# One core: attention, routed experts and a dense block. Keys read in place, logits per token, tile-by-tile scatter of expert rows

## The reference, cut to what matters

```python
# attention: B=2, H=8, S=768, D=64; blocks of 32 keys are summarised
k_sum = k.reshape(B, H, 24, 32, D).max(axis=3)
v_sum = v.reshape(B, H, 24, 32, D).mean(axis=3)
scores_l = scale * q @ k.T            # kept where |i - j| < 16, else -1e9
scores_s = scale * q @ k_sum.T + log(32)
a = softmax(concat([scores_l, scores_s]))
x = (a @ concat([v, v_sum])).reshape(1536, 512)      # token-major
# experts: w_gate (512, 8), w1 (8, 512, 1024), w2 (8, 1024, 512)
do_compute = x @ w_skip > 0
e_idx, gate_w = argmax(x @ w_gate), softmax(x @ w_gate)[e_idx]
x[do_compute] += gate_w * (relu(x @ w1[e_idx]) @ w2[e_idx])
# dense: w_in (512, 2048), w_out (2048, 512)
h = x @ w_in
out = (h * cos(h)) @ w_out
```

## Time and profile before

| | |
|---|---|
| median of 3 runs | 599.25 us (594.43 to 600.09) |
| profiled execution | 601.41 us, span 599.7 us |
| attention, to the first instruction of the routing | 0 to 152.5 us |
| routing, to the first expert product | 152.5 to 178.9 us |
| experts, to the last second product | 178.9 to 299.2 us |
| to the first dense matmul | 299.2 to 316.5 us |
| dense | 316.5 to 599.7 us |
| busy: PE, DVE, ACT, POOL | 494.9, 314.7, 217.7, 128.5 us |

### The profile page before, as it was taken

How to read it: one execution, slowest core, us unless ns; L and a number is a source line. 1 busy time by engine, 2 the same in 40 slices (tenths; PEclk the granted TensorE clock), 3 DMA queues, 4 the chain that set the end, 5 groups by cost and what they waited for, 6 DMA issues and landing times.

```text
span 599.7 us, 10654 instructions
## 1 busy us (share of the span) xinstructions
PE 494.9 (83%) x4077; PEld 384.2 (64%) x4077; DVE 314.7 (52%) x582; ACT 217.7 (36%) x522; POOL 128.5 (21%) x139
## 2 busy tenths in 40 slices
PE   2876666597168788968788988899999999999997
PEld 1665555453165456546476766678888888888885
DVE  4475565441601112111064898886777676766764
ACT  1354444363001010101062645544544444544443
POOL 6357555431033100000063313430000000000000
PEclk9978787798579889889798999999999999999999
DMA  6837888756999807077742000020400000100001
GB/s 170 208 114 230 242 263 261 210 139 204 373 404 372 323 16 290 17 304 281 292 117 99 1 0 0 2 70 2 141 0 1 1 1 0 72 0 1 1 1 70
DMA packets 48938, 79.32 MB, mean 132 GB/s; under 512 B 4345, under 2 KB 30969, under 8 KB 48890
## 3 DMA queue, kind: packets, MB, share of 16 engines
q1 hardware_dynamic: 44434, 70.68, 35.5%
q0 software_dynamic: 2080, 6.82, 3.5%
q10 hardware_dynamic: 2376, 1.18, 0.7%
HBM read 65.95 MB, written 11.14 MB: 129 GB/s over the span
## 4 chain that ended last, share of the span: by engine, by line
PE 54%; DMA 19%; DVE 11%; issue 6%; ACT 4%; SPq 3%; POOL 2%; ACTq 1%; DVEq 0%; POOLq 0%
PE bank L1133 11%; PE bank L1135 11%; PE bank L1134 11%; DMA rows_sorted<-y_out 10%; DMA v_tok<-v_pairs 5%; PE bank L1161 3%; PE bank L1058 3%; PE bank L1020 3%; PE bank L1174 3%; DVE turns L947 3%; DMA x_plain<-x_stage 2%; PE bank L1041 2%; DVE reduced L951 2%; DVE reduced L954 2%; PE bank L1140 1%
## 5 line engine op out<-in xcount | busy, mean ns | idle before, releaser
L1133 PE MATMUL bank<-wout_hi,gT_hi 128*128 128x512 f32 x192 | 76.0, 396 | 9.8 <-DVE gT_lo L966 9.8
L1133 PE MATMUL bank<-x2T,win_hi 128*128 128x512 f32 x192 | 76.4, 398 | 1.4 <-DVE x2T L934 1.4
L1134 PE MATMUL bank<-x2T,win_hi 128*128 128x512 f32 x192 | 75.3, 392 | 0.0
L1135 PE MATMUL bank<-x2T,win_lo 128*128 128x512 f32 x192 | 75.3, 392 | 0.0
L1135 PE MATMUL bank<-wout_hi,gT_lo 128*128 128x512 f32 x192 | 74.8, 390 | 0.0
L1134 PE MATMUL bank<-wout_lo,gT_hi 128*128 128x512 f32 x192 | 74.8, 390 | 0.0
L679 ACT ACTIVATE turns<-reduced,half_pi 128x512 f32<-128x512 f32 x48 | 34.7, 723 | 86.5 <-DVE reduced L957 86.5
L947 DVE TENSOR_SCALAR turns<-turns 128x512 f32<-128x512 f32 x48 | 33.0, 687 | 58.1 <-ACT turns L672 58.1
L672 ACT ACTIVATE turns<-bank,quarter 128x512 f32<-128x512 f32 x48 | 32.9, 686 | 59.1 <-PE bank L1135 59.1
L890 DVE COPY y_out<-bank 128x128 f32 x18 | 5.2, 292 | 90.8 <-PE bank L1174 57.0
L1133 PEld LDWEIGHTS bank<-wout_hi,gT_hi 128*128 128x128 f32 x192 | 36.0, 188 | 21.6 <-DVE gT_lo L966 14.4
(11 more groups left out here) (155 smaller groups left out, 863.7 us busy)
## 6 DMA issues: line engine op xcount, KB each, us to landing
w_slot<-weights SPq DMA_DIRECT2D x80, 512.0 KB, 7.0
rows_sorted<-zeros SPq DMA_DIRECT2D x7, 512.0 KB
k_padded<-k_T SPq DMA_DIRECT2D x8, 384.0 KB, 7.3
q_raw<-q_T SPq DMA_DIRECT2D x8, 384.0 KB, 4.8
v_tok<-v_pairs SPq DMA_DIRECT2D x8, 384.0 KB, 5.2
v_window<-v_pairs SPq DMA_DIRECT2D x8, 384.0 KB, 4.3
x_plain<-x_stage SPq DMA_DIRECT2D x8, 384.0 KB, 7.8
x_tile<-x_plain SPq DMA_DIRECT2D x12, 256.0 KB
```

The lines of the kernel that those rows point to most:

```text
L1133: te.matmul(out_ap, a[0], b[0], start=start, stop=False)
L1134: te.matmul(out_ap, a[0], b[1], start=False, stop=False)
L1135: return te.matmul(out_ap, a[1], b[0], start=False, stop=stop)
```

## The change

- Attention: `keys` is gone. PE multiplies each query tile by the 32 summary columns (`ksum`, L975 after) and by 96 columns of the padded keys in place (L976 after), two matmuls where there was one. `v_tok` and `q_raw` have two buffers, `k_padded` three, and SP loads them before the windows of the pair before. `place_q` works on a third of a pair behind each `normalise`; the first pair is placed by DVE. `copy_x` writes straight into `xT`; the block sums move to the head of `values`, and their copy from ACT to DVE.
- Logits: in each `transpose_x` PE adds the x block's product with the gate weights, tokens along the partitions, into one bank that collects all 12 token tiles. The stage's end has no logits matmuls, copies or transposes left.
- x is kept whole in `x_tok`: one store of half of x beside pair 5, the rest at the end. The six zero blocks are stored after the last pair's weights.
- Routing: fewer and shorter DVE steps, two of the products on ACT and POOL, and the one-hot matrix made in two halves. Added: the scatter rows, spread over four column groups by four small matmuls.
- Experts: all copies of a tile are on ACT, in one loop. POOL, once its 14 gathers are through, scatters each tile's y rows to their tokens with an indirect transfer (L517 after). `copy_y` waits for `y_free`, which POOL counts up in that same program; there are four y slots. Every four scatters use four semaphores, so a scatter waits for the one four back. SP loads expert 2's weights at the end of the attention, and two chunks of experts 3 and 4 behind each of the first eight blocks that have landed. DVE splits `w_in` during the last experts. `y` is loaded in order by SP.
- Dense: ACT makes the high part of `w_out` (two chunks ahead, six in the first group's slots 2 to 7), POOL all eight low parts. Nothing else changes.

```diff
+SLOT_OF = (0, 1, 3, 4, 2, 0, 1, 3)
...
             def load_k(i):
-                sp.dma_start(kpad[i % 2][:, WINDOW:WINDOW + S], kT[i, :, :]).then_inc(k_loaded[i % 2], 16)
+                ge(sp, scores_ready, GPP * (i - 2))
+                sp.dma_start(kpad[i % 3][:, WINDOW:WINDOW + S], kT[i, :, :]).then_inc(k_loaded[i % 3], 16)
             def load_q(i):
-                ge(sp, q_placed, i)
-                sp.dma_start(qraw[:, :], qT[i, :, :]).then_inc(q_loaded, 16)
+                ge(sp, q0_placed, min(i - 1, 1))
+                ge(sp, q_placed, GPP * (i - 2))
+                sp.dma_start(qraw[i % 2][:, :], qT[i, :, :]).then_inc(q_loaded[i % 2], 16)
             def load_vtok(i):
-                ge(sp, vs_ready, i)
-                sp.dma_start(vtok[:, :, :], v2[i, :, :].rearrange("(t p) d -> p t d", p=P)).then_inc(vtok_loaded, 16)
+                ge(sp, vs_ready, i - 1)
+                sp.dma_start(vtok[i % 2][:, :, :], v2[i, :, :].rearrange("(p t) d -> p t d", t=TPB))\
+                    .then_inc(vtok_loaded[i % 2], 16)
...
             for i in range(PAIRS):
-                sp.wait_ge(keys_ready, i + 1)
+                if i > 0 and i + 2 < PAIRS:
+                    load_k(i + 2)
                 if i + 2 < PAIRS:
-                    load_k(i + 2)
                     load_q(i + 2)
+                    load_vtok(i + 2)
                 if i > 0:
                     sp.wait_ge(xps_ready, GPP * i)
                 if i + 1 < PAIRS:
                     load_windows(i + 1)
                     place_vsum(i + 1)
-                if i + 2 < PAIRS:
-                    load_vtok(i + 2)
                 for n in range(BESIDE * i, BESIDE * (i + 1)):
                     load_chunk(n // NCH, n // NCH, n % NCH)
-                if i > 0:
-                    store_zeros(i - 1)
-                if i > 1:
-                    store_x(i - 2)
-            store_x(PAIRS - 2)
-            store_x(PAIRS - 1)
-            sp.wait_ge(xt_copied, STEPS)
-            sp.wait_ge(zero_stored, 16 * PAIRS)
-            for e in range(BESIDE, SLOTS):
-                for c in range(NCH):
-                    load_chunk(e, e, c)
+                if i == PPB + 1:
+                    store_x(GPP * PPB, 0, TPB, 0, PPB)
+            store_x(GPP * (PAIRS - 2), TPB, NT, 0, PPB - 2)
+            sp.wait_ge(zeros_ready, 1)
+            for k in range(NT // 2):
+                dst = yd[CG * P * (2 * k + NBLK):CG * P * (2 * k + NBLK + 2), :].rearrange("(p r) f -> p (r f)", p=P)
+                sp.dma_start(dst, zeros[:, :]).then_inc(zero_stored, 16)
+            store_x(GPP * (PAIRS - 1), TPB, NT, PPB - 2, PPB - 1)
+            for gr in range(GPP):
+                store_x(STEPS - GPP + gr + 1, TPB + 2 * gr, TPB + 2 * gr + 2, PPB - 1, PPB)
+            sp.wait_ge(xps_ready, STEPS)
+            for c in range(NCH):
+                load_chunk(2, SLOT_OF[2], c)
+            for k in range(NCH):
+                sp.wait_ge(blocks_ready, k + 1)
+                if k == NCH // 2:
+                    sp.wait_ge(x_stored, 16 * XSTORES)
+                    sp.wait_ge(zero_stored, 16 * (NT // 2))
+                for c in (2 * k, 2 * k + 1):
+                    load_chunk(3 + c // NCH, SLOT_OF[3 + c // NCH], c % NCH)
...
-            for done, src, s in ((1, 5, 0), (2, 6, 1), (3, 7, 2), (4, E, 3), (6, E + 1, 0)):
+            for done, src, s in ((1, 5, 0), (2, 6, 1), (3, 7, 3), (4, E, 4), (6, E + 1, 0)):
                 sp.wait_ge(expert_done, done)
                 for c in range(NCH):
                     load_chunk(src, s, c)
+            sp.wait_ge(y_all, 1)
+            for q in range(TPG):
+                load_y(q, q)
...
+            def place_q(s):
+                i, gr = s // GPP, s % GPP
+                pool.wait_ge(q_loaded[i % 2], 16 * (i // 2) + 16)
+                ge(pool, scores_ready, s - 2 * GPP + 1)
+                src = qraw[i % 2][:, GT * QT * gr:GT * QT * (gr + 1)].rearrange("p (t q) -> p t q", q=QT)
+                dst = qbd[i % 2][:, GT * gr:GT * (gr + 1), :]
+                g.tensor_scalar(dst[:, :, 0:QT], src, head_mask[:, 0:1], None, ALU.mult)
+                g.tensor_scalar(dst[:, :, QT:2 * QT], src, head_mask[:, 1:2], None, ALU.mult).then_inc(q_placed, 1)
...
+            pool.wait_ge(base_ready, 2)
+            nblocks = pool.value_load(base[0:1, E + 1:E + 2], min_val=E // CG, max_val=NBLK)
+            pool.wait_ge(idx4_ready, 1)
+            pool.wait_ge(zero_stored, 16 * (NT // 2))
+            def scatter_block(k):
+                for j in range(CG):
+                    ge(pool, y_stored[j], 16 * k)
+                    g.tensor_copy(idx_now[:, j:j + 1], idx4[:, bass.ds(k, 1), j:j + 1].rearrange("p o q -> p (o q)"))\
+                        .then_inc(idx_copied, 1)
+                    pool.sem_inc(y_free, 1)
+                    pool.wait_ge(idx_copied, CG * k + (j + 1))
+                    primed(pool, y_copied, CG * k + (j + 1))
+                    pool.sem_inc(y_taken, 1)
+                    pool.indirect_dma_start(yd, bass.IndirectOffsetOnAxis(ap=idx_now[:, j:j + 1].bitcast(U32), axis=0),
+                                            y_out[:, j, :], None).then_inc(y_stored[j], 16)
+            scatter_block(0)
+            with pool.Fori(1, nblocks) as k:
+                scatter_block(k)
+            for j in range(CG):
+                pool.wait_ge(y_stored[j], 16 * nblocks)
+            pool.sem_inc(y_all, 1)
+            for c in range(NCH):
+                pool.wait_ge(wout_hi_done, c + 1)
+                g.tensor_tensor(wout_lo[:, c, :], wslot[0][:, c, :], wout_hi[:, c, :].bitcast(F32), ALU.subtract)\
+                    .then_inc(wout_lo_done, 1)
...
+            def copy_block(n):
+                act.wait_ge(blocks_ready, n // CG + 1)
+                primed(act, t1_ready, n)
+                sc.activation(xblk[:, :], xg[:, bass.ds(n // CG, 1), :].rearrange("p o f -> p (o f)"), ACT.Copy)\
+                    .then_inc(block_copied, 1)
...
+            def copy_y(n):
+                primed(act, y_ready, n)
+                act.wait_ge(y_free, n)
+                sc.activation(y_out[:, bass.ds((n - 1) % CG, 1), :].rearrange("p o f -> p (o f)"), y_ps[:, 0:P], ACT.Copy)\
+                    .then_inc(y_copied, 1)
+            def copy_hT(n):
+                primed(act, t2_ready, n + 1)
+                primed(act, y_ready, n)
+                sc.activation(hT[:, :, :], ht_ps[:, 0:JC * P].rearrange("p (j q) -> p j q", j=JC), ACT.Copy)\
+                    .then_inc(ht_ready, 1)
+            act.wait_ge(inblk_ready, 1)
+            sc.activation(blkval[:, :, 0, :], inblk[:, :, :], ACT.Copy, scale=pcol[:, :]).then_inc(blkval_act, 1)
+            act.wait_ge(base_ready, 1)
+            ntiles = act.value_load(base[0:1, E:E + 1], min_val=E, max_val=MAXT)
+            act.wait_ge(x_stored, 16 * XSTORES)
+            copy_block(0)
+            copy_xT(0)
+            copy_block(1)
+            relu(0)
+            copy_xT(1)
+            copy_hT(0)
+            with act.Fori(1, ntiles) as n:
+                copy_block(n + 1)
+                relu(n)
                 copy_xT(n + 1)
+                copy_y(n)
+                copy_hT(n)
...
+            def copy_vs(i, par):
+                dve.wait_ge(vs_ready, i + 1)
+                ge(dve, vsum_placed, 16 * i)
+                v.tensor_copy(vs[:, :], vs_ps[par]).then_inc(vs_copied, 1)
             def copy_x(s, par):
                 dve.wait_ge(xps_ready, s + 1)
-                ge(dve, xtps_ready, s - 1)
-                ge(dve, x_kept, min(s - 1, STEPS - GPP))
-                if s == STEPS - 1:
-                    dve.wait_ge(last_kept, 1)
-                v.tensor_copy(xc[par][:, :], x_ps[par][:, 0:GT * QT]).then_inc(x_copied, 1)
+                if s % GPP == 0 and s // GPP + 1 < PAIRS:
+                    copy_vs(s // GPP + 1, par)
+                v.tensor_copy(xT[:, s // GPP, GT * QT * (s % GPP):GT * QT * (s % GPP + 1)], x_ps[par][:, 0:GT * QT])\
+                    .then_inc(x_copied, 1)
...
+            def win_high(c):
+                dve.wait_ge(w_loaded[4][c // 4], 128)
+                v.tensor_copy(win_hi[:, c, :], wslot[4][:, c, :]).then_inc(win_hi_done, 1)
+            def win_low(c):
+                dve.wait_ge(win_hi_done, c + 1)
+                v.tensor_tensor(win_lo[:, c, :], wslot[4][:, c, :], win_hi[:, c, :].bitcast(F32), ALU.subtract)\
+                    .then_inc(win_lo_done, 1)
+            dve.wait_ge(expert_done, 5)
+            win_high(0)
+            for c in range(NCH):
+                if c + 1 < NCH:
+                    win_high(c + 1)
+                win_low(c)
...
             def scores(s):
                 i, gr, par = s // GPP, s % GPP, s % 2
+                if i == 0:
+                    pe.wait_ge(q0_placed, 1)
+                ge(pe, q_placed, s - GPP + 1)
                 if gr == 0:
-                    pe.wait_ge(q_placed, i + 1)
```

(16 more changed lines are left out.)

608 lines of the change are left out of this document (232 added, 376 removed).

## The result

The changed kernel takes 577.5 us (median; 572.59 to 578.48), the kernel before 598.8: a ratio of 0.963 (95% interval 0.955 to 0.970). The forecast was 544. The profiled execution has a span of 575.5 us, 31.0 more than the 544.5 of the forecast's sum.

A forecast was written before the change was run, and what follows sets the result against it. PE was to bound the attention pair at 11.0 us, with transfers close behind; POOL's gathers, then PE, the experts. Dense starts at 263.3; 263.3 + 283.2 - 2.0 = 544.5, plus 1.7, less 2.2: 544 us, range 522 to 572.

The forecast's parts named there:

- Rival (1): Attention: transfers set the pace through the copy of `v_sum`; a pair of 12.5 us, 555 us in all; chance 0.20.
- rival (2): Experts: metered weights leave gaps, gathers take 2.0 us each, experts end 12.5 us earlier; 531 us; chance 0.18.
- (3): Attention: sums stay as late as before and a pair keeps 16 us; 574 us; chance 0.06.
- (4): Experts: scatters are served one at a time, a tile costs 13.6 us; 695 us; chance 0.03.
- of the 0.89 us of scores the 96-column part costs 96/128, 0.67 us.: Attention, each step on PE: the window part of the scores was costed by its columns, at 0.67 us.
- The 0.66 for the summary part: Attention, each step: 8 short score instructions at 0.08 us each, priced from the 9-column transposes, 0.66 us.
- so I charge 5 us: Attention: POOL's added routing constants, 4 to 7 us ahead of `normalise(7)` and `place_q(10)`, charged at 5 us.
- Now it is two steps (7.3) and one pass through the pipeline: Attention's end, last pair's scores to routing: 7.3 us of steps plus about 10 us of pipeline; routing starts at 107.1.
- 9.7 in all, which this change leaves: Experts: five PE gaps in mid-product where no engine is waited for, the longest 3.94 us, kept at 9.7 us.
- its own two savings of 3 us: Attention's start: DVE placing the first queries, and no wait for the second `v_tok`, each give about 3 us.
- the cover I named: Experts to dense: `keep_warm`, 10.68 us, hides three scatters, one landing and one load of y, about 9.5 us.
- The 40 us of gathers: Experts: 14 gathers at 2.9 us each keep their 40 us, so the y slots come free at 157.

The follow-up runs named there:

- the first run: Against the changed kernel, POOL counts `y_free` up by 4 before its gathers instead of once per slot in the first scatter block: 564.1 us, 0.940.

## Why the prediction was wrong

**Right.** The wait for `v_tok` is gone, though not by the step that the prediction named: it gave the load a pair ahead as the reason, and with one buffer and the late load the time is the same, since the later sums alone leave 9.2 us. The wait went as forecast, but by luck. PE bounds the pair, the routing is 3 us shorter (9.5 us to the first gather), the gathers keep 2.6 to 2.9 us each, `copy_y` waits for POOL once, no store of y is waited for, and dense is unchanged but for 2 us in its first group (71.7 of 77.5 us busy against 70.8 of 79.5). Rival (1), transfers in the attention, gave 12.5 us a pair for the wrong reason; rival (2) did not happen (2.6 us a gather and not 2.0), since the metering let the weights in beside the gathers all the same; when they were held back, its 2.0 us were if anything too long; (3) and (4) did not happen.

**Wrong: the sum by 31 us.** Four terms, all too low, make up 26.7 of it.

- *"of the 0.89 us of scores the 96-column part costs 96/128, 0.67 us."* This is the step that failed first. By its columns a 96-column product costs 0.17 us; it took 0.28. The scores of a step were put at 0.67 + 0.66 = 1.33 us and took 1.76. The logits took 0.47 and not 0.33, so a step without sums is 3.62 us where 3.11 was meant. Times three, with 1.43 for the sums, 12.3 a pair: 7.8 us in six pairs. The 0.66 for the summary part came out (4 x 0.17) from the transposes of the earlier trace rows, whose operand has 9 rows and not 128; that was luck. That two products cost twice one of the same columns in all is shown by the run with one product a tile; that it is the query weights loaded for each is argued, from the logits' price and from the trace, where each product has its own load of 128 x 128.
- *"so I charge 5 us"*, for POOL's constants. From the fourth scores to the last pair 9.4 us were lost, 4.4 more. 6.5 of them are the stop of 3.0 us behind the constants and the half pace after it, which went when the constants were moved. The other 2.9 are half pace behind the first stop, at 16.7 us, which the sum had at nothing; they did not go with the stop, and their cause stays open.
- *"Now it is two steps (7.3) and one pass through the pipeline"*, 17.3 us. It was 23.0. The two steps took 8.7 us, the last scores themselves, which the sum left out, 1.9 more, and the pass 12.4 where 10 were taken; by PE's timeline 1.2 of that is its last products at half pace. (The stretch that it set out from, 35.7 us before, was 29.8: 116.82 is one step too early.) Not tested by a run.
- *"9.7 in all, which this change leaves"*, for PE's gaps. From the free slots to the last second product PE took 97.8 us and not 89. The four stops are 12.1 us, 2.4 more. The half pace behind the long ones, some 3.1, I had not counted, nor the small product that the change puts behind each expert (L1119, 7 times 0.24 us = 1.7); the rest, 1.6, is not traced. Without the late weight traffic the same stretch takes 84.7 us.

The rest are small: 0.9 at the start (the prediction took the third scores for the fourth; from 25.5 its own two savings of 3 us give 19.5), 1.2 at the y slots, and 2.2 at the end, where the scatters and not the warm-up came last, so that the cover I named was 1.7 us too short:

```profile
280.33 3.81 DMA y_tokens<-y_out,row_of_slot_now
...
284.32 2.69 DMA y_stage<-y_tokens
```

The 40 us of gathers behind which y was not free, and the standstill they make, stood in the sum in full. It was seen as part of the change's price; the first run shows that it was the cheapest thing to mend.

## What to carry to other kernels

Do not cost a matmul with few columns by its columns: with weights of 128 x 128 a product took 0.22 to 0.24 us here, with 9 columns as with 128, and that it is the weight load that sets this is argued. Splitting one product of 128 columns into 32 and 96 doubled it, and reading in place was paid for on the engine that had become the bound. Before work is moved off one engine, ask which will be last afterwards, and price the move there. A stop of the matmul engine costs more than its length, and a permit that stands in an in-order program behind unrelated work is a wait, even when what it permits has been free all along.
